# Attention feeding two FFNs on one core: scores two units in front instead of one, weight chunks in four places, the later ones issued by ACT

## What is computed

```python
q_d, k_d, v_d = (mean of 4 positions of q, k, v)
out_up = np.repeat(sm_attn(q_d, k_d, v_d), factor, axis=2)
mask = np.abs(pos[:, None] - pos[None, :]) < factor
scores = np.where(mask, scale * np.matmul(q, k.transpose(0, 1, 3, 2)), -1000000000.0)
out_local = np.matmul(softmax(scores), v)
x = (out_up + out_local) as (2304, 512)
h = x @ w_in;   g = np.maximum(h, 0) + alpha * np.minimum(h, 0);   x = g @ w_out
h = x @ w2_in;  g = np.where(h > 0, h, np.exp(np.minimum(h, 0)) - 1);   out = g @ w2_out
```

## Time and profile before

| | us |
|---|---|
| median of 3 runs | 926.58 |
| lowest and highest | 925.03 and 926.87 |
| the profiled execution | 925.22 |
| its span in the trace | 923.4 |
| PE busy | 902.8 (98%) |
| DVE, ACT, POOL busy | 538.3, 300.2, 282.6 |

### The profile page before, as it was taken

The page is one execution under the profiler, slowest core; times in us unless marked ns, Lnnn a source line. Parts: engine busy times, 40 slices in busy tenths (PEclk is TensorE's granted clock), DMA queues, the critical chain, the costliest instruction groups (busy, mean ns, idle before and its releaser), DMA issues.

```text
span 923.4 us, 16942 instructions
## 1 busy us (share of the span) xinstructions
PE 902.8 (98%) x6512; PEld 836.2 (91%) x6512; DVE 538.3 (58%) x1049; ACT 300.2 (33%) x688; POOL 282.6 (31%) x406
## 2 busy tenths in 40 slices
PE   8779999999999999999999999999999999999998
PEld 5568999999999999999999998888888888988887
DVE  5636566655665554454455476656765657756563
ACT  4433334333422232232241132323442324423233
POOL 4669895111101135645566541110011100000000
PEclk9879999999999999999999999999999999999999
DMA  7555542222211123443553244434454443544411
GB/s 173 116 130 150 144 137 51 54 54 54 54 40 29 28 62 126 152 151 109 169 176 124 58 137 117 121 117 114 116 182 125 115 115 114 186 122 115 115 46 69
DMA packets 119839, 100.80 MB, mean 109 GB/s; under 512 B 66000, under 2 KB 82384, under 8 KB 119760
## 3 DMA queue, kind: packets, MB, share of 16 engines
q1 hardware_dynamic: 118576, 99.42, 38.2%
q10 hardware_dynamic: 1184, 0.30, 0.2%
HBM read 80.29 MB, written 19.40 MB: 108 GB/s over the span
## 4 chain that ended last, share of the span: by engine, by line
PE 93%; POOL 3%; issue 2%; DMA 1%; DVE 1%; SPq 0%; ACT 0%; ACTq 0%; POOLq 0%; DVEq 0%
PE ps L239 29%; PE ps L241 28%; PE ps L240 28%; PE ps L427 1%; PE ps L451 1%; PE ps L494 1%; PE ps L438 1%; PE ps L482 1%; PE ps L459 1%; PE ps L467 1%; DMA qk_nat<-in_k 1%; DMA v_nat<-in_v 1%; POOL p_l L687 1%; PE ps L447 0%; POOL p_c L684 0%
## 5 line engine op out<-in xcount | busy, mean ns | idle before, releaser
L241 PE MATMUL ps<-common,w_hi 128*128 128x384 f32 x768 | 258.8, 337 | 0.0
L240 PE MATMUL ps<-common,w_hi 128*128 128x384 f32 x768 | 258.6, 337 | 0.0
L240 PEld LDWEIGHTS ps<-common,w_hi 128*128 128x128 f32 x768 | 145.1, 189 | 0.0
L241 PEld LDWEIGHTS ps<-common,w_hi 128*128 128x128 f32 x768 | 144.7, 188 | 0.0
L239 PE MATMUL ps<-common,w_in_lo 128*128 128x384 f32 x384 | 133.3, 347 | 5.8 <-POOL w_out_lo L713 5.8
L239 PE MATMUL ps<-common,w_out_lo 128*128 128x384 f32 x384 | 132.9, 346 | 0.5 <-DVE common L318 0.5
L314 ACT ACTIVATE common<-act_g 128x384 fp32r<-128x384 f32 x96 | 50.5, 526 | 230.7 <-PE ps L241 125.3
L303 DVE TENSOR_SCALAR act_g<-ps,alpha_t 128x384 f32<-128x384 f32 x96 | 59.2, 617 | 99.1 <-PE ps L241 99.1
L865 ACT ACTIVATE act_g<-act_g 128x384 f32<-128x384 f32 x96 | 50.5, 526 | 195.0 <-DVE act_g L861 195.0
L239 PE MATMUL ps<-w_hi,common 128*128 128x512 f32 x288 | 113.6, 394 | 0.0
L241 PE MATMUL ps<-w_hi,common 128*128 128x512 f32 x288 | 113.5, 394 | 0.0
(11 more groups left out here) (100 smaller groups left out, 1464.7 us busy)
## 6 DMA issues: line engine op xcount, KB each, us to landing
ring<-w_in_parts SPq DMA_DIRECT2D x168, 256.0 KB, 2.7
w_in_parts<-parts SPq DMA_DIRECT2D x8, 1280.0 KB, 5.8
qk_nat<-in_q SPq DMA_DIRECT2D x32, 144.0 KB, 2.8
v_nat<-in_v SPq DMA_DIRECT2D x16, 288.0 KB
out<-xT SPq DMA_DIRECT2D x18, 256.0 KB, 2.2
qk_nat<-in_k SPq DMA_DIRECT2D x30, 144.0 KB, 3.1
v_win<-in_v SPq DMA_DIRECT2D x64, 67.5 KB
xT<-in_moe_w_in SPq DMA_DIRECT2D x16, 256.0 KB, 2.9
```

The costliest lines, as they stand in the source:

```text
L240: pe.matmul(psum, l_hi, r_lo, start=False, stop=False)
L241: return pe.matmul(psum, l_hi, r_hi, start=False, stop=stop)
```

## The change

- Scores run two units in front and R three. The prologue holds R and scores of units 0 and 1 and R of unit 2. Step u does TC(u), TL(u), SC and SL of u+2, R of u+3, O(u).
- The probabilities and their stats have two places, by u % 2, and the waits on their readers go back two units. The sums and reciprocals of unit u+2 are now made at O(u) in all steps.
- On POOL step u is sum_v(u), one split (two chunks on each side of sum_v from step 4 on), normalise(u+2), instead of normalise(u+1), sum_v(u+1), split.
- Four places for chunks, in the region of the last two batches of xT; SP loads chunks 0 to 3 in the prologue and steps 0 to 2, and ACT issues the load of chunk c+4 behind g_hi of chunk c in the first tile.
- SP loads q and k of u+4 in step u; in the prologue v_nat(0) comes behind k(1), v_win(0) and chunk 0 ahead of q(3) and k(3).
- Fillers of the prologue: 9, 5 and 6 instead of 9, 5 and 10.

```diff
-    AHEAD_OF = {"TC": 0, "TL": 0, "O": 0, "SC": 1, "SL": 1, "R": 2}
+    AHEAD_OF = {"TC": 0, "TL": 0, "O": 0, "SC": 2, "SL": 2, "R": 3}
...
-    prologue = [(*job, 0) for job in ROUNDS + FIRST_SCORES] + [(*job, 1) for job in ROUNDS]
+    prologue = [(*job, u) for u in range(2) for job in ROUNDS + FIRST_SCORES] + [(*job, 2) for job in ROUNDS]
...
-        WS = 2
+        WS = 4
...
-            p_c, p_l = sb("p_c", [QM, CB, SD]), sb("p_l", [QM, NW, KP])
+            p_cs, p_ls = sb("p_cs", [QM, 2, CB, SD]), sb("p_ls", [QM, 2, NW, KP])
...
                 elif kind == "O":
                     if i == 0:
-                        if BATCH_UNITS <= u and u + 1 < UNITS:
-                            if u + 2 == UNITS:
-                                sum_local(dve, u + 1, 0)
-                            sum_local(dve, u + 1, 1)
-                            reciprocals(dve, u + 1)
+                        if u + 2 < UNITS:
+                            if u + 3 == UNITS:
+                                sum_local(dve, u + 2, 0)
+                            sum_local(dve, u + 2, 1)
+                            reciprocals(dve, u + 2)
                         copy_coarse(dve, u)
...
-            w_stage = xT[:, (B - 1) * NXB:B * NXB, :, :].rearrange("p w k q -> p (w k q)")[:, 0:WS * CH]\
+            w_stage = xT[:, (B - 2) * NXB:B * NXB, :, :].rearrange("p w k q -> p (w k q)")[:, 0:WS * CH]\
...
+                    if u + 4 < UNITS:
+                        sp.wait_ge(r_done, 4 * (u + 3) + 2)
+                        load_q(sp, u + 4)
+                        sp.wait_ge(r_done, 4 * (u + 3) + 4)
+                        load_k(sp, u + 4)
+                    if u + 1 < WS:
+                        load_chunk(sp, u + 1)
                     if u + 1 < UNITS:
                         sp.wait_ge(o_done, 2 * (u + 1))
                         load_v_windows(sp, u + 1)
...
+                    if job == ("SL", 0, 1):
+                        keep_busy(6)
...
-                keep_busy(10)
...
                         if what == "hi":
                             g_hi_part(act, t, at)
+                            if t == 0 and at + WS < FC:
+                                load_chunk(act, at + WS)
...
-                            if at[1:] == ("O", 0, UNITS - PAIRS):
+                            if at[1:] == ("O", 0, UNITS - 2 * PAIRS):
                                 dve.wait_ge(w_split, FC)
...
                 normalise(gp, 0)
+                normalise(gp, 1)
                 for u in range(BATCH_UNITS):
-                    normalise(gp, u + 1)
-                    sum_v(gp, u + 1)
+                    if u:
+                        sum_v(gp, u)
                     split_weights(gp, u // 2, u % 2)
+                    normalise(gp, u + 2)
```

More of the change, by code:

```diff
@@ L114, in bank_of @@
             return i + 2 * (kind == "TL")
-        if u == 0 and kind in ("SC", "SL"):
+        if u < 2 and kind in ("SC", "SL"):
             return 4 + {("SL", 0): 0, ("SL", 1): 1, ("SC", 0): 2}[kind, i]
-        step, place = (u - 1, SCORES.index((kind, i))) if kind in ("SC", "SL") else (u, OUTPUTS.index((kind, i)) + 1)
+        step, place = (u - 2, SCORES.index((kind, i))) if kind in ("SC", "SL") else (u, OUTPUTS.index((kind, i)) + 1)
         return 4 + (step + place) % 3
@@ L342, in attention_then_two_ffns @@
             qd, kdT = sb("qd", [P, SD + HR - QW]), sb("kdT", [P, SD])
[L343 removed]
+            p_cs, p_ls = sb("p_cs", [QM, 2, CB, SD]), sb("p_ls", [QM, 2, NW, KP])
             pT_c, pT_l = sb("pT_c", [SC, 2, HEADS, SD]), sb("pT_l", [2 * KP, NWH, HEADS, QW])
[L345 to L347 removed]
+            stats = sb("stats", [QM, 2, 3, NST])
+            coarse_bias = sb("coarse_bias", [QM, CB])
             coarse_o = sb("coarse_o", [P, SD])
@@ L353, in attention_then_two_ffns, with p_c, p_l, maxes @@
             dense = xT[:, NXB:NXB + 2, :, :].bitcast(BF16).rearrange("p w k q -> p (w k q)")
+            def p_c(u):
+                return p_cs[:, u % 2, :, :]
+            def p_l(u):
+                return p_ls[:, u % 2, :, :]
+            def maxes(u, columns=slice(0, NST)):
+                return stats[:, u % 2, 0, columns]
+            def sums(u, columns=slice(0, NST)):
+                return stats[:, u % 2, 1, columns]
+            def recips(u, columns=slice(0, NST)):
+                return stats[:, u % 2, 2, columns]
             def slots(g):
@@ L650, in dve_job @@
                 elif kind == "R":
-                    if u < BATCH_UNITS + 2 and i < 2:
-                        sum_local(dve, u - 1, i)
-                        if i == 1:
-                            reciprocals(dve, u - 1)
                     pool_round(dve, u, i)
-                    if u >= BATCH_UNITS + 2 and i == 1:
+                    if i == 1:
                         sum_local(dve, u - 1, 0)
@@ L943, in _, with step_loads @@
             def _(sp):
-                def step_loads(u, chunks, late_chunks):
+                def step_loads(u):
                     if u + 1 < UNITS:
@@ L1102, in _ @@
                     copy_round(act, 0, r)
-                for g in range(2):
-                    exp_local(act, 0, g)
-                exp_coarse(act, 0)
-                for r in range(4):
-                    copy_round(act, 1, r)
+                for u in range(2):
+                    for g in range(2):
+                        exp_local(act, u, g)
+                        for r in (2 * g, 2 * g + 1):
+                            copy_round(act, u + 1, r)
+                    exp_coarse(act, u)
                 for u in range(BATCH_UNITS):
@@ L1202, in _ @@
                 dve.memset(xT[:, NXB:NXB + 2, :, :], 1.0).then_inc(dense_set, 1)
-                dve.memset(sums[:, :], 1.0).then_inc(ones_set, 1)
+                dve.memset(stats[:, :, :, :], 1.0).then_inc(ones_set, 1)
                 dve.memset(qd[:, SD:], 0.0).then_inc(padded, 1)
-                dve.memset(p_l[:, :, KW:KP], 0.0).then_inc(padded, 1)
+                dve.memset(p_ls[:, :, :, KW:KP], 0.0).then_inc(padded, 1)
                 for r in range(4):
                     pool_round(dve, 0, r)
-                for g in range(2):
-                    subtract_max(dve, 0, g)
-                max_coarse(dve, 0)
-                dve.wait_ge(ones_set, 1)
-                for g in range(2):
-                    sum_local(dve, 0, g)
-                reciprocals(dve, 0)
-                for r in range(4):
-                    pool_round(dve, 1, r)
+                for u in range(2):
+                    for g in range(2):
+                        subtract_max(dve, u, g)
+                    max_coarse(dve, u)
+                    for r in range(4):
+                        pool_round(dve, u + 1, r)
+                    if u == 0:
+                        dve.wait_ge(ones_set, 1)
+                    for g in range(2):
+                        sum_local(dve, u, g)
+                    reciprocals(dve, u)
                 for u in range(BATCH_UNITS):
@@ L1313, in _ @@
                 normalise(gp, 0)
+                normalise(gp, 1)
                 for u in range(BATCH_UNITS):
-                    normalise(gp, u + 1)
-                    sum_v(gp, u + 1)
+                    if u:
+                        sum_v(gp, u)
                     split_weights(gp, u // 2, u % 2)
+                    normalise(gp, u + 2)
                 for u in range(BATCH_UNITS, UNITS):
-                    for c in LATE[u - BATCH_UNITS] if u < 2 * BATCH_UNITS else ():
+                    late = LATE[u - BATCH_UNITS] if u < 2 * BATCH_UNITS else ()
+                    for c in late[:2]:
                         for which in range(2):
                             split_weights(gp, c, which)
-                    if u + 1 < UNITS:
-                        normalise(gp, u + 1)
-                        sum_v(gp, u + 1)
+                    sum_v(gp, u)
+                    for c in late[2:]:
+                        for which in range(2):
+                            split_weights(gp, c, which)
+                    if u + 2 < UNITS:
+                        normalise(gp, u + 2)
                 gp.wait_ge(x_done, 2 * UNITS)
```

108 lines of the change are left out of this document (46 added, 62 removed).

## The result

The changed kernel takes 910.87 us (median of 4 runs, 910.17 to 912.40), the kernel before 926.03 us (median of 4, 925.03 to 926.87). The ratio is 0.984, 95% interval 0.982 to 0.986: 15.2 us less, where the forecast had 16.6 (926.6 to 910.0). The total came out; one of its three terms (B, the attention stage) was well short in the profiled run.

The account below looks back on a forecast made before the run. PE, full from 80 us on, bounds the kernel, so time could be won only in the first 80 us or by removing later PE work. A 7.2, B 4.9 and C 3.5 sum to 15.6 us, giving 910 us (905.5 to 915).

Parts of the forecast that it names:

- B: Attention stage up to the FFN's first product: first product at 50.5 instead of 55.43 us, 4.9 us won.
- A: Start of the FFN, first product to unit 4's coarse output: split wait and slow stretch go, 7.2 us (5.8 to 8.0).
- The fourth quarter of x: Start of the FFN: the next thing late, ending 4.1 us after the first product starts, just covered by PE work.
- C: PE-saturated part: one unit's scores and transposes move ahead of the first product, 3.5 us off the end (3.3 to 3.8).
- step 0 ends at 26.5: Attention stage, end of the first step: 24.4 us plus 2 us of waiting for k of unit 3 (24.4 to 28).
- the 8.0 us for a step: Attention steps 1 to 3: length set near transfers and the loop on the single v_win, bounds 7.4 and 9.3 us.
- D: Edits costed at nothing: ACT's 12 chunk loads, POOL's sum_v behind two splits, later split waits; 0.5 to 1 us if failing.
- (1): Attention steps stay about 10.2 us through transfers and SP's queue; first product at 58.7, total 917.8; chance 0.12.
- (2): Whole kernel: everything closes up and the clock stays up, 20.5 us won, total 904.7; chance 0.12.
- (3): FFN chunk loads come too late, PE stalls per chunk, 928 or more; slack 8.6 us for chunk 7; chance 0.03.

Follow-up runs that it names:

- e3: Changed kernel with the load of alpha moved from the prologue to behind v_win(3) in step 2: 913.39 us, ratio 0.987 to the kernel before.
- e4: Changed kernel with 8 filler matmuls in step 0 ahead of R of unit 3: 911.69 us, ratio 0.985 to the kernel before.
- e5: Changed kernel with SP loading only chunk 1 in step 1, and chunks 2 and 3 in step 3: 909.57 us, ratio 0.983 to the kernel before.
- e9: Changed kernel with SP loading weight chunk 0 behind q and k of unit 3 instead of ahead: 910.60 us, ratio 0.984 to the kernel before.
- e10: Changed kernel with chunk 0 behind q and k of unit 3, chunks 2 and 3 in step 3, alpha at the head of step 3: 911.10 us, ratio 0.984.
- e12: Changed kernel with chunks 2 and 3 loaded in step 3 and six fillers ahead of unit 3's q/k transposes: 909.80 us, ratio 0.983.
- e11: Changed kernel run again without any edit: 910.70 us (910.24 to 916.73), ratio 0.985 to the kernel before.
- e8: Changed kernel with VectorE, in steps 0 to 3, copying coarse output and writing x before unit u+2's sums and reciprocals: 915.27 us, ratio 0.990.
- e2: Kernel before with four places for weight chunks and nothing else, SP still issuing every chunk: 921.49 us, ratio 0.996.
- e6: Changed kernel with only two places for weight chunks, all issued by SP and none by ACT: 924.50 us, ratio 0.998 to the kernel before.
- e7: Changed kernel with ACT asking for chunk c where it has made g of chunk c-2, two chunks later: 933.31 us, ratio 1.007 to the kernel before.
- e1: Kernel before with POOL, in step 3, doing the last half of chunk 1's split ahead of normalise(4) and sum_v(4): 920.18 us, ratio 0.994.

## Why the prediction was right, and where it was not

**A, right.** Forecast 7.2 us (5.8 to 8.0), measured 26.23 - 18.17 = 8.1 us, just past the bound, and 7.5 to 7.9 in e3, e4, e5, e9, e10 and e12. I had 19.0 us for the stretch; eight of the nine profiles with the change's four places and its order on POOL and DVE (all but e11, where the clock fell) have 18.1 to 18.7. The parts: 5.9 us for the wait, 1.9 for the slow stretch behind it, where I had 1.4 (from the tenth matmul to the end of unit 4's transposes 4.52 us before, 2.64 after), and 0.3 by a shorter wait for DVE's part of g (0.54 before, 0.23 now). The fourth quarter of x, for which I left nothing, cost nothing: PE has no wait between 54.48 and 62.47.

**C, right.** Forecast 3.5 us (3.3 to 3.8), measured 841.74 - 837.95 = 3.8 us. Six variants (e4, e5, e8 to e10, e12) and the repeat have 837.94 to 838.04, so this term is as firm as any number here. e2, without the lead, has 841.80: the term belongs to the lead.

**B, over-estimated.** Forecast 4.9 us (-0.5 to 8.7), measured 55.43 - 54.48 = 0.95 in the profiled run. That run is longer than the others; with A and C as firm as above, the medians leave 15.2 - 7.7 - 3.8 = 3.7 us for B (worked out, not seen in a profile of the changed kernel; the profiles of variants with 1.7 us of clock missing have 51.0 to 53.2, thus 2.3 to 4.4 us). The first step that failed is "I take 2 us of waiting: step 0 ends at 26.5". It ended at 29.08. The waits for q and k of unit 3 were 2.78 us, not 2, and the slow clock behind them cost another 1.5 (from the k transposes to TC 4.20 us, where e3 and e4, at clock 1.00, have 2.65) and 1.4 more in step 1, read above; I had put a price on the wait and none here on the clock that falls after it. The second is the 8.0 us for a step. The mean of steps 1 to 3 is 8.5, and e5's 8.2; the size was near, the reason was in the main not the one I gave. I named transfers and v_win. v_win is one wait of 1.12 us, the last of step 3. Step 1 is long by slow clock alone, and steps 2 and 3 wait for DVE's write of x (1.03, 0.55 us), which the coarse scores of two units on need for their bank. I had counted DVE as busy time of a step (6.7 us, and it is 6.78) and not as a loop with PE of 7.87 us.

**D, right at its size, wrong in its reason.** PE has no wait behind 69 us, so ACT's 12 loads cost nothing. But e6 shows that places and queue don't only relieve SP in the attention stage: without them the lead gains 0.9 us and not 15.2, since POOL's later sum_v holds up SP's queue, and the chunks with it. I had treated "POOL's sum_v now stands behind two chunk splits" as a line of D without cost and did not ask who waits behind it.

**Rivals.** (1) Steps of 10.2 us: one step of e9, e10 and e3 is that long (10.4, 10.2 and 10.3), behind a late transfer, and two of e8 behind vd, but never the mean. Its sign, a first product past 56 us, stands in e11 (56.10) with the clock as the cause. (2) Everything closing up, 904.7: its A and C came true, its B in no run; the lowest time of all is 907.65, of e5. (3) Chunks late: its slack was real but smaller, 5 us for chunk 4 where I had 6 to 8, and e7 shows the price beyond it, 22 us.

**The sum.** 8.1 + 0.95 + 3.8 = 12.8 us is the profiled difference (925.2 to 912.4) where I had 15.6: B is 4.0 short and A and C are 1.2 over. At the medians 15.2 us: B is 1.2 us short, A and C are 0.8 over, within the ranges given. So part of the good total is that errors of opposite sign met. And 15.6 us off the median of 926.6 are 911.0, not the 910 that I wrote, which came from the shorter profiled run.

**Parts against the whole.** Each against the kernel before as it ran beside it: POOL's order alone gives 5.9 us (926.12 to 920.18), four places alone 4.6 (926.12 to 921.49), the lead with POOL's order, without places and ACT's queue, 0.9 (925.36 to 924.50). The second and the third make up the whole between them (but for who issues the late chunks), and give 5.5 us where the whole gives 15.2. Each part alone runs into the wait that another removes: e1 waits for p_c, which only the lead cures; e2 keeps the 5.78 us for the split; e6 waits for chunks.

## What to carry to other kernels

When a loop of engines is taken away in a stage where the DMA engines are already near 1.00, ask which transfer is late next: here a step that ended earlier was followed by a wait for the next one (e3, e4, e9), and the medians show nothing won. Look too for a loop between two engines that are both far from full: DVE and PE, busy 6.78 and 6.86 us, set a step of 7.87. Price a wait of TensorE together with the slow clock behind it, 1 to 3 us in these profiles. When a job is moved back on one engine, follow the queue that waits for it to the last thing in it: v_nat's load waited for sum_v, and a weight chunk stood behind v_nat.

## What the runs showed that was not expected

**The same wait, another clock.** The two profiles of the changed kernel have waits of 1.12 and 1.15 us in front of the same local output. In one the granted clock stays at 1.00, in the other it is 0.71 over the 10 us around it (part of them at the 1.2 GHz level) and 0.95 over the next. The two runs are 4.3 us apart. The mean clock of a run sorts its time: in both sets of the changed kernel 910.2 to 911.3 us at 0.998, 912.4 and 912.6 at 0.996, 916.7 at 0.990. Why it falls in one run and not in the other after equal waits is open.

**Two us behind the last matmul.** e3 is 1.9 us longer in its rest than the others, all of it at the end. The last matmul of the change, then the last matmul of e3 and a row of its DMA queues from 903 to 912 us, which the change doesn't have in that window:

```profile
907.12 0.40 PE L241 MATMUL ps<-w_hi,common 128*128 128x512 f32 x1
```

```profile
905.82 0.40 PE L241 MATMUL ps<-w_hi,common 128*128 128x512 f32 x1
...
q8 instruction: 1, 0.02, 1.0%
```

From the last matmul to the end of the span are 3.5 us in the one and 5.4 in the other, and e3 has a fetch of instructions (queue q8) there. It isn't one fetch more: both have 53 packets on q8, and the last one is 9 us before the end of the span in the change (901.6 to 902.6), ahead of the last output, and 4 us before it in e3 (907.2 to 908.2), in the midst of the output. Behind it e3's queues still move a few packets for 2 us. That moving one DMA in the first 50 us should move a fetch at the end, I can't explain, and that the fetch is what holds up the end is not shown. All four runs of e3 are long (912.97 to 914.16), so it isn't one run's accident.
